# Block-causal attention and two feed-forward layers: query and key rows that hold both heads, masks copied by ScalarE, and 17 products that nothing reads

## What is computed

```
scores = (q @ k^T) / 8          # 32 heads, [576, 576]
scores = where(block(i) >= block(j), scores, -1e9)   # blocks of 64
attn = softmax(scores)          # e / (sum(e) + 1e-9)
x = attn @ v                    # [2304, 512]
for alpha in (1, 1.702):
    h = x @ w_in                # [2304, 2048]
    x = (h * sigmoid(alpha * h)) @ w_out
```

## Time and profile before

| | us |
|---|---|
| median of 3 runs | 948.2 (948.01 to 948.34) |
| the profiled execution | 947.78 |
| its span, first to last instruction | 946.0 |
| TensorE busy in the span | 928.8 (98%) |
| VectorE, ScalarE, GpSimd busy | 528.2, 384.5, 299.6 |

### The profile page before, as it was taken

How to read it: one execution, slowest core, us unless ns; L and a number is a source line. 1 busy time by engine, 2 the same in 40 slices (tenths; PEclk the granted TensorE clock), 3 DMA queues, 4 the chain that set the end, 5 groups by cost and what they waited for, 6 DMA issues and landing times.

```text
span 946.0 us, 14419 instructions
## 1 busy us (share of the span) xinstructions
PE 928.8 (98%) x5304; PEld 795.0 (84%) x5304; DVE 528.2 (56%) x1096; ACT 384.5 (41%) x854; POOL 299.6 (32%) x408
## 2 busy tenths in 40 slices
PE   5999999999999999999999999999999999999998
PEld 4888877787778777877788889999999999999997
DVE  6777756565657556655445435454654455644443
ACT  4677634453435434543323323232433233523222
POOL 6899337653554354435717200000000000000000
PEclk9999999999999999999999999999999999999999
DMA  9555695795788764888537986434364534364431
GB/s 267 168 149 159 184 315 175 232 326 179 220 268 263 245 195 137 267 268 272 181 116 279 360 314 210 125 111 131 104 191 110 134 102 132 107 195 104 131 102 67
DMA packets 65190, 179.57 MB, mean 190 GB/s; under 512 B 7136, under 2 KB 8800, under 8 KB 59232
## 3 DMA queue, kind: packets, MB, share of 16 engines
q1 hardware_dynamic: 64688, 177.99, 59.8%
q10 hardware_dynamic: 432, 0.66, 0.2%
HBM read 130.02 MB, written 44.56 MB: 185 GB/s over the span
## 4 chain that ended last, share of the span: by engine, by line
PE 94%; DVE 1%; POOL 1%; ACT 1%; issue 0%; POOLq 0%
PE ps_y L967 20%; PE ps_y L1025 13%; PE ps_a L1026 7%; PE ps_h L950 7%; PE ps_h L952 6%; PE ps_h L951 6%; PE ps_a L929 5%; PE ps_a L917 4%; PE ps_a L998 4%; PE ps_a L1001 4%; PE ps_a L1000 4%; PE ps_h L998 3%; PE ps_h L1001 3%; PE ps_h L1000 3%; PE ps_a L869 2%; PE ps_a L897 2%
## 5 line engine op out<-in xcount | busy, mean ns | idle before, releaser
L967 PE MATMUL ps_y<-g_hi,w_hl 128*128 128x512 f32 (+1 forms) x640 | 189.1, 378 | 0.0
L1025 PE MATMUL ps_y<-o_hi,w_out 128*128 128x512 f32 x368 | 139.9, 391 | 0.0
L967 PEld LDWEIGHTS ps_y<-g_hi,w_hl 128*128 128x128 f32 x640 | 112.0, 189 | 16.6 <-DVE g_lo L1376 0.4
L967 PE MATMUL ps_y<-g_lo,w_hl 128*128 128x512 f32 (+1 forms) x320 | 118.5, 370 | 0.0
L1152 ACT ACTIVATE g_f<-ps_h 128x512 f32<-128x512 f32 (+1 forms) x71 | 40.8, 575 | 189.2 <-PE ps_h L952 189.2
L950 PE MATMUL ps_h<-x_hi,w_hl 128*128 128x512 f32 (+1 forms) x284 | 111.6, 393 | 0.2 <-POOL w_hl L750 0.2
L1371 DVE SCALAR_TENSOR_TENSOR g_f<-g_f,ps_h 128x512 f32<-128x512 f32 x63 | 43.3, 688 | 117.8 <-ACT g_f L1152 117.4
L952 PE MATMUL ps_h<-x_lo,w_hl 128*128 128x512 f32 (+1 forms) x284 | 107.7, 379 | 0.0
L951 PE MATMUL ps_h<-x_hi,w_hl 128*128 128x512 f32 (+1 forms) x284 | 107.2, 377 | 0.0
L1026 PE MATMUL ps_a<-o_hi,w_out 128*128 128x256 f32 x368 | 103.0, 280 | 0.0
L1133 ACT ACTIVATE p_sb<-ps_a,nmax 128x512 f32<-128x512 f32 (+4 forms) x128 | 72.3, 572 | 67.0 <-DVE nmax L1340 66.5
(11 more groups left out here) (151 smaller groups left out, 1899.3 us busy)
## 6 DMA issues: line engine op xcount, KB each, us to landing
w_form<-f_split SPq DMA_DIRECT2D x168, 256.0 KB, 2.7
w_hl<-w_split SPq DMA_DIRECT2D x30, 1024.0 KB, 7.5
w_raw<-w_chunks SPq DMA_DIRECT2D x42, 512.0 KB, 5.7
w_split<-w_hl SPq DMA_DIRECT2D x16, 1024.0 KB, 7.8
f_split<-stage SPq DMA_DIRECT2D x24, 512.0 KB, 5.7
o_split<-stage SPq DMA_DIRECT2D x16, 512.0 KB, 4.1
w_out<-o_split SPq DMA_DIRECT2D x16, 512.0 KB, 7.5
k_raw<-kT SPq DMA_DIRECT2D x28, 288.0 KB, 5.9
```

The source lines that it names most:

```text
L967: last = nc.tensor.matmul(bank_y(t, k), lhs, rhs, start=(part == 0 and f == 0 and (t > 0 or k % 2 == 0)), stop=(part == 2 and f == NF - 1) ...
L1025: nc.tensor.matmul(y_main(k), lhs, rhs[:, h, 0:512], start=begin, stop=end, skip_group_check=True)
```

## The change

Four edits.

1. The host lays queries and keys out by depth (`by_depth`), so that one partition's row holds both heads: one piece of 4096 bytes for queries and of 4608 for keys, where there were two. The tiles on the chip are as before.
2. `place_masks` goes from SyncE, where it was four DMAs ahead of `load_v(0)`, to ScalarE, where it is four copies ahead of `early_exp(0)`. TensorE's wait on them counts to 4.
3. `invert` adds 1e-9 to the two sums of a unit in one instruction. There are 64 units.
4. TensorE makes 6 products of `ident` with itself ahead of the first scores and 11 between the scores and the transposes, into a bank whose contents nothing reads. Its wait for `ident` moves to the front.

```diff
+WARM = (6, 11)
...
                 for half in range(2):
-                    sp.dma_start(raw(n)[0][D * half:D * half + D, :, :],
-                                 qT[n, :, :].rearrange("(h d) c -> d h c", h=2)).then_inc(s_q[n % 2], 16)
+                    sp.dma_start(raw(n)[0][D * half:D * half + D, :, :].rearrange("d h c -> d (h c)"),
+                                 qT[n, :, :]).then_inc(s_q[n % 2], 16)
...
-            def place_masks():
-                sp.wait_ge(s_mask, 8)
-                for h in range(2):
-                    sp.dma_start(q_mask[D:P, h, :].bitcast(F32), mask_q[D:P, :]).then_inc(s_maskd, 16)
-                    sp.dma_start(k_mask[D:P, h, :].bitcast(F32), mask_k[D:P, :]).then_inc(s_maskd, 16)
...
-            place_masks()
...
-                        pe.wait_ge(s_maskd, 64)
+                        pe.wait_ge(s_maskd, 4)
...
+            def warm(n):
+
+                for _ in range(n):
+                    nc.tensor.matmul(bank(1)[:, 0:P], ident[:, :], ident[:, :], start=True, stop=True, skip_group_check=True)
+
+            pe.wait_ge(s_ident, 2)
+            warm(WARM[0])
             early_scores(0)
             early_scores(1)
-            pe.wait_ge(s_ident, 2)
+            warm(WARM[1])
             early_transposes(0)
...
+            def place_masks():
+                act.wait_ge(s_mask, 8)
+                for h in range(2):
+                    nc.scalar.activation(q_mask[D:P, h, :], mask_q[D:P, :], ACT.Copy).then_inc(s_maskd, 1)
+                    nc.scalar.activation(k_mask[D:P, h, :], mask_k[D:P, :], ACT.Copy).then_inc(s_maskd, 1)
...
+            place_masks()
             early_exp(0)
...
-                nc.vector.tensor_scalar(den_e[:, a:a + 1], den[:, a:a + 1], 1e-9, None, ALU.add)
-                nc.vector.tensor_scalar(den_e[:, b:b + 1], den[:, b:b + 1], 1e-9, None, ALU.add).then_inc(s_den, 1)
+                nc.vector.tensor_scalar(den_e[:, a:b + 1], den[:, a:b + 1], 1e-9, None, ALU.add).then_inc(s_den, 1)
...
+    def by_depth(a):
+
+        return a.reshape(JOBS, 2, D, -1).transpose(0, 2, 1, 3).reshape(JOBS, D, -1)
...
-        "qT": qp[:, :, BLK:],
-        "kT": kp,
+        "qT": by_depth(qp[:, :, BLK:]),
+        "kT": by_depth(kp),
```

More of the change, by code:

```diff
@@ L533, in load_keys @@
                 for half in range(2):
-                    sp.dma_start(raw(n)[1][D * half:D * half + D, :, :],
-                                 kT[n, :, :].rearrange("(h d) c -> d h c", h=2)).then_inc(s_k[n % 2], 16)
+                    sp.dma_start(raw(n)[1][D * half:D * half + D, :, :].rearrange("d h c -> d (h c)"),
+                                 kT[n, :, :]).then_inc(s_k[n % 2], 16)
             def copy_keys(n):
```

## The result

The changed kernel took 950.97 us at the median of 9 runs, the kernel before 948.28 of 9 on the same chip: ratio 1.0025, 95% interval 1.0015 to 1.0035, slower. A second set, taken at the end of the experiments, gave 949.48 beside 948.66 (11 and 21 runs): 1.0004, 0.9995 to 1.0013. Over both sets the means are 950.05 and 948.64, so 0.15% slower; the forecast was 0.12% faster.

The account below looks back on a forecast made before the run. TensorE bounds the kernel, busy throughout 100 to 300 us, with room only in the first 100. 0.75 + 0.14 + 0.17 = 1.06 us off 947.78 gives 946.7; the median lies 0.4 above, 947.1 us; range 945.6 to 948.5.

Parts of the forecast that it names:

- The level: Opening: products raise TensorE's clock between 7 and 11.5 us, transposes take 0.60 us for 1.11, `hidden` earlier; 0.75 us gained.
- a rival: Opening: level rises before 7 us, 946.7 us; chance 0.3 shared with faster longer rows or both.
- All that follows until 25 us ... moves with it: After `hidden`'s start, a chain of waits until 25 us was to shift by the same 0.75 us.
- The premise that scores alone do not raise the level: Opening: before, scores of 3.7 us with 3.5 us idle behind them did not raise the clock.
- The products' own length: TensorE's opening: 0.43 us per 128-column product at the lower level, 0.21 at the higher; six take 2.6 us.
- They cost TensorE time where it idles: Opening: six products end near 4.1 us, before 4.99, costing nothing; eleven end between 10.9 and 13.2, transposes due at 12.24.
- One addition: VectorE's `invert`: one addition for two saves 0.07 us at each of two waits for exponentials, 0.14 us.
- the waits for exponentials at 25 and 69 us that might grow: Sign of being wrong: TensorE's waits there grow because VectorE and GpSimd meet at other points; no size given.
- Masks: Copies hidden in ScalarE's idle time; GpSimd gets chunk 3 earlier, TensorE's wait at 39.60 us goes, 0.17 us gained.
- Longer rows: Transfers of queries and keys to 64 partitions: rate stays about 231 GB/s, gain 0.
- The slower side: Over 0.2% slower, above 950.1 us: no mechanism priced, chance 0.04; the rival on this side was 948.6 us.
- late transposes: Rival in the opening: level rises only after the transposes, which start 1.0 us late; 948.6 us, chance 0.1.

Follow-up runs that it names:

- only_rows: The kernel before with only the longer one-piece rows of queries and keys; ratio 0.9999 (0.9991 to 1.0008).
- only_masks: The kernel before with only the four mask copies moved from SyncE's DMAs to ScalarE; ratio 0.9998 (0.9989 to 1.0007).
- tiny: The kernel before plus the 17 products at the same places, each over 4 columns in place of 128; ratio 1.0015 (1.0006 to 1.0024).
- only_warm: The kernel before with only the 17 products nothing reads; ratio 1.0022 (1.0014 to 1.0031).
- warm_wide: The kernel before plus the 17 products' columns (768 and 1408) in 5 products of 384 or 512; ratio 0.9996 (0.9987 to 1.0004).
- keep: The kernel before plus 6 and 10 unread products ahead of the scores of job 0's second and third unit; ratio 1.0000 (0.9992 to 1.0009).
- no_add: The kernel before without any addition of 1e-9, reciprocals taken of the sums themselves; ratio 0.9999 (0.9991 to 1.0008).
- one_reduce: The kernel before with one sum over pairs (tensor_reduce) per unit in place of the two additions; ratio 0.9995 (0.9986 to 1.0004).
- only_invert: The kernel before with only the single addition over 128x2 ahead of each reciprocal; ratio 1.0011 (1.0001 to 1.0020).

## Why the prediction was wrong

- **The level (0.75 us)** was right as a mechanism: it rose, even at 4.70 us, which was a rival; transposes at 0.66 us; `hidden` at 18.00 with the products alone. The rule that transposes do not get the full clock ("TensorE: Matmul & The Clock Gate" of the Trainium skill, Part 4, PE-mode transpose) did not hold here either: four took 0.66 us at 10.91. Two steps failed. "All that follows until 25 us ... moves with it": what was late next was the keys' transfer, for which ScalarE waited 1.6 to 1.9 us in each of the four profiles with the 17 products and no mask DMAs; that brought job 0's `ends` back to 16.96, where before's began at 16.83. And I let the level stay up: it fell at 14.94 us while TensorE waited between the transposes and `hidden`, and the `ends` took 2.15 us for 1.47, so that `hidden` came at 19.46. In place of 0.75 us gained, that profile shows 0.87 lost, of which up to 0.8 can be the chance of the level's rise. The premise that scores alone do not raise the level held for the one profile I had, not for the kernel: in `only_rows` and `only_masks`, with the same scores, it was up for 3.4 us at 8 to 12 us.
- **The products' own length** came out short, without effect: 3.68 us for 16 pairs are 0.23 us, not 0.21, and a product of 128 columns took 0.49 us at the lower level (2.93 for six) and 0.25 at the higher, where I had 0.43 and 0.21.
- **"They cost TensorE time where it idles"** priced the products as work, and left out that they are instructions to be loaded. This is the larger failure: 0.15 to 0.22% where the products stand alone (`tiny`, `only_warm`). That the instructions cost it, and not their columns, is shown by `tiny` against `warm_wide`; that their packets do is argued from the traces.
- **One addition (0.14 us)**: "128x1 takes 0.15 and I expect no more than 0.02 above it". It took 0.258 in the mean and 1.04 at most, and alone made the kernel 0.1% slower. The text itself named the place, the waits for exponentials at 25 and 69 us that might grow (2.4 us at 26.6, 1.8 before), but as a doubt without a price.
- **Masks**: right. Four copies hidden on ScalarE from 4.8 to 6.9 us, GpSimd's cast of 26.67 us at 25.65 in `only_masks` (forecast 25.2), TensorE's wait for GpSimd at 39.6 us gone. The 0.17 us itself can't be told: 0.9998.
- **Longer rows (0)**: right. 246 and 238 GB/s at 8.5 to 11.5 us beside 231, `only_rows` at 0.9999.
- **The slower side**: its mechanism, late transposes, did not occur; they began 1.3 us earlier. Its 0.04 for over 0.2% slower had no term for transfers that collide or engines that lock each other out, though the earlier trace rows showed a transfer on the path.

Theory P (the port) is shown by a pair of kernels that differ in that instruction, and by the times at which the long additions end. Theory I (instruction packets) is weaker: `tiny` and `warm_wide` differ in instructions and in weight loads, no run moved a packet by itself, and the packets at 12 to 14 us do not explain chunk 1. The sizes do not add up: products and addition alone cost 0.22 and 0.11%; the whole with the sum over pairs, which has all 17 products, their packet at 92.3 us and the queries at 6.73, stands at 1.0002, the whole with the wide products at 1.0002 too, and the whole itself at 1.0025 and 1.0004. That the masks' edit takes away the wait at 41 us is a part of it. With intervals of about 0.1% on each side the rest stays open.

## What to carry to other kernels

Before joining small instructions on VectorE, ask whether the joined form takes the ports it shares with GpSimd: a longer reciprocal or reduction does not, an addition of a number over two columns does, and the profile tells by its maximum, not its minimum. Work that nothing reads is still instructions: use few wide products, and look where the instruction queue's packets then fall among the transfers that somebody waits for. If run times of one kernel lie in two groups, read the granted clock of each run before explaining a difference of 0.1%, and before a shift of under 1 us in one profile is explained, look how far two profiles of the same program lie apart there.

## What was new of the hardware

- A transfer of 512 KB landed 1.0 us later in the profiles with a 16 KB instruction packet inside it (7.05 against 6.01 in the mean of 9 and 11, no overlap). That the packet is the cause is not shown by itself.
- An addition of a number over 128x2 in fp32 can be held until a running GpSimd instruction ends: 18 to 24 of 64 took over 250 ns, up to 1.05 us; over 128x1 (157 ns at most), a reciprocal over 128x2 (168) and a sum over pairs (158) do not.
- By the mean clock, before's granted clock fell for 3.4 us in 43% of its runs, 1.6 us each; filling TensorE's idle time at 20 to 25 us took that to 1 of 12. The same opening of TensorE's program met the rise of the level at 17.0 to 17.6 us in some executions (before, `keep`, `no_add`) and at 20.0 to 20.1 in others (`one_reduce`, `only_invert`).
